# Attention scores from split queries and keys in one-pass products, and one weight chunk per attention block

## The reference, cut to what matters

```python
# attention: batch 2, heads 8, seq 768, head_dim 64, n_sink 4, window 128
scores = (1/8) * q @ k.T                       # float32
keep   = (key < n_sink) | ((query - key >= 0) & (query - key < window))
scores = where(keep, scores, -1e9) - rowmax
a      = exp(scores) / (sum(exp(scores)) + 1e-9)
x      = (a @ v)  -> (1536, 512)
# layer 1: 8 experts, top 2 per token, w1 (8, 512, 1024), w2 (8, 1024, 512)
x = sum over the two chosen experts of weight * relu(x @ w1[e]) @ w2[e]
# layer 2: 8 experts, the best one per token, same sizes
x = gate * relu(x @ w1b[e]) @ w2b[e]
```

## Time and profile before

| | us |
|---|---|
| three runs | 676.68, 676.58, 675.33 |
| their median | 676.58 |
| profiled execution | 674.08 |
| its span | 672.0 |
| end of attention (last sink product starts) | 129.06 |
| TensorE busy | 639.0 (95%) |
| DVE busy | 329.8 (49%) |
| ACT busy | 275.7 (41%) |
| GpSimd busy | 184.7 (27%) |

### The profile page before, as it was taken

How to read it: one execution, slowest core, us unless ns; L and a number is a source line. 1 busy time by engine, 2 the same in 40 slices (tenths; PEclk the granted TensorE clock), 3 DMA queues, 4 the chain that set the end, 5 groups by cost and what they waited for, 6 DMA issues and landing times.

```text
span 672.0 us, 11238 instructions
## 1 busy us (share of the span) xinstructions
PE 639.0 (95%) x3866; PEld 580.1 (86%) x3867; DVE 329.8 (49%) x681; ACT 275.7 (41%) x529; POOL 184.7 (27%) x199
## 2 busy tenths in 40 slices
PE   7989999899999999999999999999988999999981
PEld 6989999898999999999999999988767888788871
DVE  4466645588365526254361634467876222542220
ACT  5667866442344335252443523144516123522110
POOL 2500100117362533516144251201652121121010
PEclk9999999999999999999999999999998999999996
DMA  7867822263684646646355520724649211001000
GB/s 209 281 235 240 291 74 80 66 249 74 237 214 138 132 148 157 190 142 156 111 122 177 148 28 3 171 63 159 171 138 387 102 48 47 20 32 48 16 32 11
DMA packets 51089, 89.84 MB, mean 134 GB/s; under 512 B 7919, under 2 KB 14063, under 8 KB 51040
## 3 DMA queue, kind: packets, MB, share of 16 engines
q1 hardware_dynamic: 41872, 69.21, 31.0%
q0 software_dynamic: 9168, 19.97, 13.3%
HBM read 73.13 MB, written 17.02 MB: 134 GB/s over the span
## 4 chain that ended last, share of the span: by engine, by line
PE 82%; DVE 6%; DMA 3%; ACT 3%; issue 2%; SPq 1%; ACTq 0%; POOL 0%; DVEq 0%; POOLq 0%
PE banks L1060 6%; PE banks L1059 6%; PE banks L999 6%; PE banks L1078 6%; PE banks L1001 6%; PE banks L998 6%; PE banks L803 5%; PE banks L831 4%; PE banks L1377 3%; PE banks L1342 3%; PE banks L1347 3%; PE banks L1343 3%; PE banks L1373 3%; PE banks L1374 3%; PE banks L815 2%
## 5 line engine op out<-in xcount | busy, mean ns | idle before, releaser
L1833 DVE TENSOR_TENSOR split<-stage,split 128x2048 fp32r<-128x2048 f32 x32 | 73.3, 2290 | 41.9 <-ACT split L1463 41.8
L998 PE MATMUL banks<-xTs,split 128*128 128x416 f32 (+1 forms) x256 | 88.6, 350 | 0.0
L999 PE MATMUL banks<-xTs,split 128*128 128x416 f32 (+1 forms) x256 | 86.5, 342 | 0.0
L650 POOL DMA_INDIRECT x_moe<-rows,dst_idx x25 | 49.3, 1971 | 113.2 <-DVE rows L2285 112.2
L1059 PE MATMUL banks<-hTs,split 128*128 128x416 f32 x224 | 79.9, 357 | 0.0
L1060 PE MATMUL banks<-hTs,split 128*128 128x416 f32 x224 | 78.6, 351 | 0.0
L1598 ACT ACTIVATE hTs<-banks 128x416 fp32r<-128x416 f32 x56 | 29.0, 518 | 81.6 <-PE banks L1001 81.6
L1463 ACT ACTIVATE split<-stage 128x2048 fp32r<-128x2048 f32 x32 | 60.9, 1908 | 1.0 <-DMA stage<-w1a 1.0
L1720 ACT ACTIVATE hTs<-banks 128x512 fp32r<-128x512 f32 x28 | 16.5, 596 | 105.8 <-PE banks L1357 105.8
L1001 PE MATMUL banks<-xTs,split 128*128 128x416 f32 (+1 forms) x256 | 56.2, 340 | 0.0
L803 PE MATMUL banks<-k_sb,q_sb 128*128 128x260 f32 (+2 forms) x192 | 49.6, 384 | 3.5 <-DMA k_sb<-k_w 2.1
(11 more groups left out here) (371 smaller groups left out, 1308.3 us busy)
## 6 DMA issues: line engine op xcount, KB each, us to landing
stage<-w1a SPq DMA_DIRECT2D x16, 1024.0 KB, 7.6
stage<-w2a SPq DMA_DIRECT2D x16, 1024.0 KB, 5.4
k_sb<-k_w SPq DMA_DIRECT2D x12, 520.0 KB, 5.0
raw<-w1b SPq DMA_DIRECT2D x4, 1024.0 KB, 7.9
raw<-w2b SPq DMA_DIRECT2D x4, 1024.0 KB, 9.7
q_sb<-q_t SPq DMA_DIRECT2D x24, 128.0 KB, 3.1
x_attention<-rows SPq DMA_DIRECT2D x12, 256.0 KB, 6.1
split<-x_moe SPq DMA_DIRECT2D x12, 256.0 KB, 3.6
```

Of the source, the lines that this page charges most:

```text
L650: pool.indirect_dma_start(out=x_dram[1], out_offset=rows_at(dst_idx[0], early_dst, e, k), in_=y_lines(e, k), in_offset=None, compute_op=AL ...
L998: pe.matmul(psum, piece(slot, 0, o + c * FH), xTs[:, 0, c, 0:cols], start=(c == 0), stop=False)
L999: pe.matmul(psum, piece(slot, 1, o + c * FH), xTs[:, 0, c, 0:cols], start=False, stop=False)
L1833: dve.tensor_tensor(split_chunk(e % 2, 1, c), staged_chunk(e % 2, c), split_chunk(e % 2, 0, c).bitcast(F32), ALU.subtract).then_inc(low_do ...
```

## The change

Queries and keys are split into high and low parts, and a score becomes two one-pass products instead of a float32 one. The head dimension is 64, so 64 partitions hold the high parts of the keys of one head and the other 64 their low parts. The query is held twice, once for each half of the partitions. `q_high` times this stack gives high times high plus high times low, and `q_low` times it gives the rest.

Keys are loaded and split once: a ring (`k_ring`, one per batch) holds two blocks and the sink keys, and block i writes slot i % 2. The order of the columns then changes with the block's parity, so there is a fourth mask, and `transposes`, `values` and `pack_sinks` take other offsets. DVE splits the keys (`split_keys`: two copies and two subtractions per pair of head pairs). In block 0 it does so at every step, for blocks 0 and 1; later at each odd step for the block that follows. GpSimd splits the queries (`split_queries`: a copy and a subtraction), those of block 1 before and those of block 2 behind the selects on v, later four times per block. Block 0 keeps the float32 scores. SP loads a unit once its raw buffers have been split. The chunks of expert 0 are loaded and split one per block, in blocks 2 to 5.

```diff
+            q_high = sb_early("q_high", [P, BATCH, 2, PAIRS, P], F32R)
+            q_low = sb_early("q_low", [P, BATCH, 2, PAIRS, P], F32R)
+            q_raw = sb_early("q_raw", [P, BATCH, 2, PAIRS, P])
+            k_raw = sb_early("k_raw", [P, BATCH, PAIRS, P])
...
+                if i == 1:
+                    sp.wait_ge(scores_ready, 4 * b + 1)
+                else:
+                    sp.wait_ge(k_split, keys_split(i - 1, b, 1))
+                    sp.wait_ge(q_split, queries_split(i - 1, b, 1))
+                sp.dma_start(k_raw[:, b], k_unit[:, :, P:2 * P]).then_inc(qk_in[b], 16)
+                for twice in range(2):
+                    sp.dma_start(q_raw[twice * HD:(twice + 1) * HD, b].rearrange("p h j n -> p h (j n)"),
+                                 q_unit.rearrange("(h p) j n -> p h (j n)", h=2)).then_inc(qk_in[b], 16)
...
-            for i in (1, 2):
+            for i in range(1, BLOCKS):
                 for b in range(BATCH):
+                    if i + 1 < BLOCKS:
+                        load_unit(i + 1, b)
                     store_x(i - 1, b)
...
+                if i <= CHUNKS:
+                    load_first(sp, 0, i - 1)
+                if i > 2:
+                    zero_rows(4 * (i - 3), 4 * (i - 2) + (i == BLOCKS - 1))
...
+            def split_queries(i, b, g):
+                pairs = slice(2 * g, 2 * g + 2)
+                if g == 0:
+                    pool.wait_ge(qk_in[b], 48 * (i + 1))
+                if i > 1:
+                    pool.wait_ge(scores_ready, (i - 1) * 8 + 4 * b + 2 * g + 2)
+                pool.tensor_copy(q_high[:, b, :, pairs, :], q_raw[:, b, :, pairs, :]).then_inc(q_split, 1)
+                pool.wait_ge(q_split, queries_split(i, b, g) - 1)
+                pool.tensor_tensor(q_low[:, b, :, pairs, :], q_raw[:, b, :, pairs, :], q_high[:, b, :, pairs, :].bitcast(F32),
+                                   ALU.subtract).then_inc(q_split, 1)
...
+            split_all_queries(1)
+            pool.wait_ge(vs_in, 16 * BATCH)
...
+            split_all_queries(2)
...
             for i in range(2, BLOCKS - 1):
-                for b in range(BATCH):
-                    pack_sinks(i, b)
+                split_queries(i + 1, 0, 0)
+                pack_sinks(i, 0)
+                split_queries(i + 1, 0, 1)
+                split_queries(i + 1, 1, 0)
+                pack_sinks(i, 1)
+                split_queries(i + 1, 1, 1)
...
-                    mm = pe.matmul(S[:, j % 2, h, 0:n], q_sb[:, b, pair, h, :], k_sb[:, b, pair, 0:n], start=True, stop=True)
+                    if kind == 0:
+                        mm = pe.matmul(S[:, j % 2, h, 0:P], q_first[:, b, pair, h, :], k_first[:, b, pair, :], start=True, stop=True)
+                    else:
+                        keys, psum = k_ring[b][:, h, pair, 0:WIN], S[:, j % 2, h, 0:WIN]
...
+                        pe.matmul(psum, q_high[:, b, h, pair, :], keys, start=True, stop=False)
+                        mm = pe.matmul(psum, q_low[:, b, h, pair, :], keys, start=False, stop=True)
...
+            def split_keys(i, b, g):
+                o, pairs = slot_of(i), slice(2 * g, 2 * g + 2)
+                raw_keys = k_raw[:, b, pairs, :] if i else k_first[:, b, pairs, :]
+                if i > 0 and g == 0:
+                    dve.wait_ge(qk_in[b], 48 * (i + 1))
+                half = (slice(0, HD), slice(HD, P))
+                for h in range(2):
+                    link(dve.tensor_copy(k_ring[b][half[h], h, pairs, o:o + P], raw_keys[half[h]]))
+                for h in range(2):
+                    dve.tensor_tensor(k_ring[b][half[1 - h], h, pairs, o:o + P], raw_keys[half[h]],
+                                      k_ring[b][half[h], h, pairs, o:o + P].bitcast(F32), ALU.subtract).then_inc(k_split, 1)
...
+                    if i == 0:
+                        if j < 4:
+                            split_keys(0, j // 2, j % 2)
+                        else:
+                            split_keys(1, (j - 4) // 2, j % 2)
+                        if j == 3:
+                            for n in range(BATCH):
+                                sink_keys(n)
+                    elif j % 2 and not last:
+                        split_keys(i + 1, j // 4, j // 2 % 2)
+                    if j in chunks:
+                        first_layer_low(0, chunks[j])
...
-            block_steps(2, 2, 2, (0, 1))
-            block_steps(3, 2, 2, (2, 3))
-            block_steps(4, 2, 2)
+            block_steps(2, 2, 2, {2: 0})
+            block_steps(3, 2, 2, {2: 1})
+            block_steps(4, 2, 2, {2: 2})
...
-            block_steps(BLOCKS - 1, 2, None)
+            block_steps(BLOCKS - 1, 2, None, {7: 3})
```

More of the change, by code:

```diff
@@ L21 @@
 WIN = 2 * P + SINK
+ODD = P + SINK
+RING = 2 * ODD
 PAIRS = HEADS // 2
@@ new lines, in _ @@
+            pool.wait_ge(setup_ready, 2)
+            select(ident[:], 0, 1, [[-1, P]], 1.0, setup_ready, ALU.not_equal)
+            select(masks[:, 1, SINK:P], SINK - 1, -1, [[1, P - SINK]], MASKED, setup_ready)
+            select(masks[:, 1, P:2 * P], 0, 1, [[-1, P]], MASKED, setup_ready)
+            for odd in range(2):
+                select(masks[:, 2 + odd, ODD * (1 - odd):ODD * (1 - odd) + P], -1, -1, [[1, P]], MASKED, setup_ready)
+                select(masks[:, 2 + odd, ODD * odd:ODD * odd + P], 0, 1, [[-1, P]], MASKED, setup_ready)
@@ L1525, in block_steps @@
                         x_copy(*((i, 0) if b else (i - 1, 1)))
-                    if pair == 0 and b < len(chunks):
-                        first_layer_high(0, chunks[b])
+                    if j in chunks:
+                        first_layer_high(0, chunks[j])
             act.preload_act_table_set("natural_log_exp_and_others")
```

127 lines of the change are left out of this document (65 added, 62 removed).

## The result

| | before | after |
|---|---|---|
| median, us | 676.16 (675.33 to 676.68, 4 runs) | 710.99 (706.37 to 715.32, 4 runs) |
| profiled execution, us | 674.08 | 712.23 (span 710.5) |
| last sink product of attention, us | 129.06 | 164.77 |

The changed kernel takes 1.0515 times as long (95% interval 1.0445 to 1.0585), 35 us more. The forecast was 684.6 us, 8 more, in a range of 664 to 694: the sign was right and the size wrong. In the two profiles most of the difference is attention: its last sink product comes 35.7 us later, and what follows takes 545.7 us against 542.9.

What follows compares the result with a forecast made beforehand. Attention was taken as TensorE's, with DVE pacing blocks 0 and 1 after the change. Block 2's mask 11.6 us late, -2.7 in blocks 2 to 4, -0.9 in block 5: +8.0, so 684.6 us, range 664 to 694.

Steps and rivals of the forecast that it cites:

- TensorE's gain: Score products in attention: 0.42 us less per pair of heads, at most 16.8 us over five blocks.
- DVE's and GpSimd's prices: Cost of one split group: 1.4 us on DVE for keys, 1.8 us with its wait on GpSimd for queries.
- The collisions: DVE copies and subtractions delayed by GpSimd: 7 us (block 0), 3 (block 1), 2.7 per block (2 to 4).
- Block 0: DVE sets the pace with 16.8 us of work from 9.0 us, ending 4.0 late, plus 7 of collisions.
- Blocks 1 to 4: DVE's summed work sets the length: 17.9 us plus collisions, 3 in block 1; blocks 2 to 4 20.6 each.
- the wait ahead of block 2: TensorE's first scores of block 2 stand behind DVE's last v row: about 1.0 us.
- at the lower clock: Block 0, all operations colliding: TensorE's 1.1 us of work per step at 1.2 GHz about DVE's step, nothing added.
- Block 5: Four score pairs save 1.7 us, chunk 3's subtraction ahead of the last `sink_lows` loses 0.8: -0.9 us.
- the first: Collisions are rare in attention, blocks 2 to 4 at 18.3 us: -8.9, 667.5 us; chance 0.25.
- second: TensorE sets attention's pace throughout, even in block 0: about 660 us; chance 0.06.
- fourth: Half the collisions in attention: 673 to 679 us; chance 0.13.
- The third: All operations collide, block 0 +14 us, blocks 2 to 4 at 21.8: +19.6, 696 us; chance 0.06.

Runs made afterwards that it cites:

- e_old_products: Changed kernel with all its splitting, but one float32 product a head for the scores as before the change: 709.31 us, ratio 1.0482.
- e_no_selects: Changed kernel without GpSimd's eight selects on the sink rows of v: 706.02 us, ratio 1.0388.
- e_late_wait: Changed kernel with TensorE's wait for the sink rows of v moved from before block 2 to before the first sink product: 700.55 us, ratio 1.0394.
- e_neither: Changed kernel with queries (on ScalarE) and keys (on DVE) only rounded, low parts left zero: 685.46 us, ratio 1.0103.
- e_nopool_gap_fill: Changed kernel with ScalarE rounding queries, no GpSimd splitting, and idle products in fewer pieces at TensorE's long waits: 688.58 us, ratio 1.0139.
- gap_fill_again: Changed kernel with idle products only at TensorE's long waits, nothing left out, a repeat run: 710.06 us, ratio 1.0461.
- after_again: Changed kernel, unchanged, measured a second time: 712.56 us, ratio 1.0510.
- e_nopool: Changed kernel without GpSimd's query splitting; ScalarE rounds the queries, their low parts stay zero: 695.65 us, ratio 1.0248.
- e_best: Changed kernel; ScalarE rounds queries, GpSimd only subtracts, idle products at TensorE's long waits, sink-row wait moved to the first sink product: 690.25 us, ratio 1.0235.
- b_small: Kernel before, block 0 loading only 128 key columns and TensorE's sink-row wait moved to the first sink product: 679.45 us, ratio 1.0019.
- e_nopool_fill: Changed kernel with ScalarE rounding queries, no GpSimd splitting, and idle products in every step and before sink products: 702.23 us, ratio 1.0339.

## Why the prediction was wrong

**TensorE's gain**: right in kind, too large by a seventh. Products stand 0.12 us apart, but a pair takes 0.56 us (0.48 only behind a sink product) where before it took 0.87 to 0.96, so about 0.365 us less on average and not 0.42: some 14.6 us over five blocks and not 16.8. And nothing of it can be seen in the time (`e_old_products`).

**DVE's and GpSimd's prices**: two terms too small. A free split group has the forecast operations, 0.61 + 0.87 us (2 x 0.30 + 2 x 0.43), but from its start to the next instruction it takes 1.54; the parts in the prediction add up to 1.52, and it went on with 1.4. GpSimd's copy takes 0.61 (0.66), its subtraction 1.27 where I had 1.05, so its group is 1.95 us and not 1.8.

**The collisions**: right in kind, near in sum, partly by luck. Over attention DVE's copies and subtractions took 16.7 us more than free ones (medians 0.291, 0.421 and, for sink keys, 0.178 us): 21.5 - 40 x 0.291 = 9.9, 21.2 - 40 x 0.421 = 4.4, block 0's own keys 1.6, sink keys 0.9. I had 7 + 3 + 3 x 2.7 = 18.1 in all, but 7 in block 0, where 9.6 were lost, and 3 and 2.7 in the others, where it was 2.1, 2.0, 2.0 and 1.1: there only copies met GpSimd, and every subtraction kept its 0.42 us. By the Trainium skill (SBUF — State Buffer, Who interferes with whom) all four operations of a group are open to it, and the trace agrees: a pair of copies lost up to 1.3 us (25.16), a pair of subtractions up to 1.9 (21.98), while the masks beside them kept their 0.28 and 0.42. GpSimd loses as well: its 20 copies took 916 ns on average, 615 in the median.

**Block 0**: here the step failed by a size. DVE's instructions follow each other from 8.65 to 36.09 us: 17.8 us of own work, where I had 16.8 (eight groups at 1.54 and not 1.4), and 9.6 of collisions in four groups and the sink keys (14.99 to 34), where I took 7, since POOL ran without a pause from 15.05 to 33.1. That is the 27.4; forecast were 23.8. GpSimd's selects, which I had counted among its 17 us, are 4.0 us of the block (`e_no_selects`).

**Blocks 1 to 4**: the step that failed. It set a block's length to the sum of DVE's work, "20.6 us each" for blocks 2 to 4. DVE's work came out below that, 18.1 to 18.8, and the blocks took 25.8 to 27.6. The same holds for block 1: DVE 19.97 of work, forecast 20.9, length 27.14. Of that, 4.16 us are the wait ahead of block 2, which the prediction put at "about 1.0": a collided group of DVE (58.17) stands in front of the last row of v. `e_late_wait` gives 8 us for it by the medians, more than its length; the clock that falls behind it (0.80 in 60 to 63 us) may be the rest, which is not shown. In the place of that step the runs show a stack, for a block of 2 to 4:

- 20.3 to 20.7 with the rounding alone, at 0.93 to 1.00 (`e_neither`). I had 18.3 for a block of DVE's 17.9 without collisions (and 17.8 for TensorE, 18.3 by the measured pair), so next to nothing for the chain of scores, mask, exponential, transposes, copy and values through four queues.
- 21.2 to 21.9 with the keys' splitting, at 0.92 to 1.00 (`e_nopool_gap_fill`).
- 22.9 to 23.2 with GpSimd's too, at 1.00 (`gap_fill_again`).
- 24.2 to 27.6 as they are, at 0.93 to 0.77 (after and `after_again`).

The last step is what the prediction denied: "at the lower clock (1.2 GHz) its 1.1 us of work per step would still be about DVE's step, so I add nothing". I said this of block 0 alone, and for the other blocks I did not ask what follows when TensorE idles 2 to 3 us in each, which I had forecast myself (3.1 to 4.4 in the rows). How much of the 35 us the clock is stays open: 2.5 us by the medians of one chip, which is not clear of their spread, 3.6 by the ends of attention there, 4.8 to 5.5 in one block of `e_nopool` and 7 between the medians of `e_nopool` and `e_nopool_gap_fill`. The idle products take time themselves, so these are what is left after paying for them. For block 0 the sentence held, since DVE set its length.

**Block 5**: -0.9 forecast, +0.3 measured (21.91 against 21.59); chunk 3's price was 0.7 to 1.2 (forecast 0.8), so the saving of the four pairs did not come. (`after_again` has 21.55, so 0.4 us between two profiles is no more than their spread.)

**Rivals**: the first, second and fourth (collisions rare, TensorE the pace, half the collisions: 667.5, 660, 673 to 679) are refuted by the time and by the same rows; the first one's own sum gives 667.7. The third (all collide, 696) had a sum nearer to the result by the wrong route: not all collided.

So by the ratios, of the 35 us some 10 to 12 are the keys' low parts (5.5 us lost to GpSimd's selects are among them), 8 GpSimd's splitting with its collisions, 10 to 11 appear only with both, and 4 to 7 are the rest. The part that appears only with both is as uncertain as it is large, and what it consists of is open. The wait ahead of block 2 and the low clock run through all four, and were not separated from each.

## What to carry to other kernels

When an engine's work is taken from a full TensorE and given to engines with room, the block's length is not the largest of the new sums: price the steps' chain from a run in which nothing is full, and ask of each new wait of TensorE whether it lowers the clock, since then the work saved is paid back at half speed. Two engines that both split data in SBUF and are released by the same event met in each of blocks 0 to 4 here. Taking the rounding off GpSimd gave back 12 us and asking for one wait later 8; splitting the keys a step earlier gave nothing. An order in which the two never meet was not tried.

## What the runs showed that I had not expected

- A wait on gathered rows some 30 us after attention (first layer for the rest of the tokens) is 0.4 us in the profile of before, 3.5 in after's, and 7.2 and 2.0 in the two profiled side by side:

```profile
PE banks L1227 <- issue: 7.2, 1, 7.2
...
PE banks L1236 <- DVE xTs_rest L2358: 2.0, 1, 2.0
```

  The stretch from the last sink product to the end of the span took 541.3 (`e_best`) to 551.7 us (`e_no_selects`), with the same code, and 542.9 and 549.4 in before and `b_small`. What makes the gather late was not found. It is why the end of attention and the median can disagree by 5 us, and why changes of 1 us could not be told here.
- 128x512 bfloat16 products meant as idle work are not free even where they keep the clock up: two to six per step and four at each sink product cost 6.6 us in `e_nopool_fill`; in fewer pieces, at the waits alone, 7 us were gained (`e_nopool_gap_fill`).
- GpSimd's subtraction of 512 elements per partition takes 1.27 us and its copy 0.61, the 1024-element select 1.14: the subtraction costs twice the copy's time per element.
